# Splitting w_out only in the first tile of each MLP and fetching the split parts from DRAM afterwards

## What is computed

```
x = attention(q, k, v)           # 8 heads of 64; each row sees 96 local and 8 global keys
h = x @ w_in;  g = h * cos(h);   x = g @ w_out          # MLP 1, d_ff 2048
h = relu(x @ w_in2);             out = (h * h) @ w_out2  # MLP 2, d_ff 2048
```

## Time and profile before

| | before |
|---|---|
| device time, median of 3 | 1246.7 us |
| device time of the profiled execution | 1248.4 us |
| its span, first to last instruction | 1246.6 us |
| TensorE busy | 1218.5 us (98%) |
| DVE busy | 736.8 us (59%) |
| ACT busy | 559.6 us (45%) |
| Pool busy | 625.1 us (50%) |
| DMA packets | 118.8 MB, 32.6% of the 16 engines' time |
| granted TensorE clock | 0.999 |

### The profile page before, as it was taken

The page is one execution under the profiler, slowest core; times in us unless marked ns, Lnnn a source line. Parts: engine busy times, 40 slices in busy tenths (PEclk is TensorE's granted clock), DMA queues, the critical chain, the costliest instruction groups (busy, mean ns, idle before and its releaser), DMA issues.

```text
span 1246.6 us, 18120 instructions
## 1 busy us (share of the span) xinstructions
PE 1218.5 (98%) x6240; PEld 991.6 (80%) x6240; DVE 736.8 (59%) x1434; ACT 559.6 (45%) x1164; POOL 625.1 (50%) x687
## 2 busy tenths in 40 slices
PE   5789999999999999999999999999999999999998
PEld 3667888887888877888888888888888888888887
DVE  6579988888878888788888933223323223223222
ACT  4656767666666666676433322222222222222211
POOL 4468966555666665666543433333334334333332
PEclk9999999999999999999999999999999999999999
DMA  4523434333433333342155441131131221311211
GB/s 122 146 70 102 110 101 137 97 89 92 146 97 104 124 89 104 112 133 84 54 148 177 138 138 52 51 111 51 51 116 46 81 89 49 113 51 51 78 50 60
DMA packets 150949, 118.80 MB, mean 95 GB/s; under 512 B 63680, under 2 KB 115008, under 8 KB 150848
## 3 DMA queue, kind: packets, MB, share of 16 engines
q1 hardware_dynamic: 150848, 117.55, 32.6%
HBM read 96.54 MB, written 20.97 MB: 94 GB/s over the span
## 4 chain that ended last, share of the span: by engine, by line
PE 94%; DVE 2%; ACT 1%; POOL 1%; DMA 1%; issue 1%; SPq 0%; DVEq 0%; ACTq 0%; POOLq 0%
PE psum L557 14%; PE psum L559 14%; PE psum L558 14%; PE psum L576 8%; PE psum L582 7%; PE psum L583 7%; PE psum L581 7%; PE psum L578 7%; PE psum L577 7%; PE psum L651 3%; PE psum L615 3%; PE psum L636 2%; PE psum L593 1%; ACT probs L771 1%; POOL probs L487 0%
## 5 line engine op out<-in xcount | busy, mean ns | idle before, releaser
L472 POOL TENSOR_SCALAR w_out_hi<-w_out_raw 128x512 fp32r<-128x512 f32 x192 | 136.5, 711 | 549.8 <-PE psum L583 312.6
L557 PE MATMUL psum<-x_parts,w_in_hi 128*128 128x512 f32 x768 | 302.9, 394 | 2.6 <-ACT hs L800 2.6
L559 PE MATMUL psum<-x_parts,w_in_lo 128*128 128x512 f32 x768 | 299.4, 390 | 0.0
L558 PE MATMUL psum<-x_parts,w_in_hi 128*128 128x512 f32 x768 | 298.8, 389 | 0.0
L474 POOL TENSOR_TENSOR w_out_lo<-w_out_raw,w_out_hi 128x512 fp32r<-128x512 f32 x192 | 264.2, 1376 | 16.0
L1017 DVE TENSOR_TENSOR g_lo<-act_a,g_hi 128x512 fp32r<-128x512 f32 x192 | 139.9, 729 | 187.1 <-ACT g_hi L812 181.7
L802 ACT ACTIVATE hs<-psum 128x512 f32<-128x512 f32 x96 | 57.4, 598 | 359.9 <-PE psum L559 359.9
L557 PEld LDWEIGHTS psum<-x_parts,w_in_hi 128*128 128x128 f32 x768 | 144.2, 188 | 32.0 <-issue 3.6
L559 PEld LDWEIGHTS psum<-x_parts,w_in_lo 128*128 128x128 f32 x768 | 144.2, 188 | 30.6
L558 PEld LDWEIGHTS psum<-x_parts,w_in_hi 128*128 128x128 f32 x768 | 144.4, 188 | 28.9
L576 PE MATMUL psum<-g_hi,w_out_hi 128*128 128x512 f32 x384 | 157.7, 411 | 0.5 <-issue 0.5
(11 more groups left out here) (76 smaller groups left out, 1657.6 us busy)
## 6 DMA issues: line engine op xcount, KB each, us to landing
w_out_raw<-in_moe_w_out_dram SPq DMA_DIRECT2D x192, 256.0 KB, 2.7
vals<-in_v_dram SPq DMA_DIRECT2D x80, 112.0 KB
w_stage<-in_moe_w_in_dram SPq DMA_DIRECT2D x32, 256.0 KB, 3.0
w_dram<-w_stage SPq DMA_DIRECT2D x16, 512.0 KB, 3.3
raw<-in_k_dram SPq DMA_DIRECT2D x96, 64.0 KB, 2.5
raw<-in_q_dram SPq DMA_DIRECT2D x96, 64.0 KB, 2.3
y_dram<-y_stage SPq DMA_DIRECT2D x24, 256.0 KB, 3.7
x_raw<-y_dram SPq DMA_DIRECT2D x6, 1024.0 KB, 5.1
```

The lines of the kernel that those rows point to most:

```text
L472: pool.tensor_scalar(hi, row, 1.0, 1.0, ALU.mult, ALU.mult).then_inc(w_out_hi_ready, 1)
L557: pe.matmul(to, hi, x[:, 0, c], start=(c == 0), stop=False)
L558: pe.matmul(to, hi, x[:, 1, c], start=False, stop=False)
L559: last = pe.matmul(to, lo, x[:, 0, c], start=False, stop=(c == KC - 1))
```

## The change

The parts of `w_out` become one tensor, hi and lo side by side. Pool splits a chunk only where `is_split(F)` is true, which is in steps 0 to 15 and 96 to 111, the first tile of each MLP. SP then stores the two parts (512 KB) in the new `w_out_dram`, and in the other 160 steps fetches them from there by one DMA of 512 KB. `split_out(F)` gets one more condition: the buffer that it writes, that of step F - 3, must have been stored.

```diff
+    w_out_dram = nc.dram_tensor("w_out_dram", (2, FC, P, 2, DM), F32, kind="Internal").ap()
...
-            w_out_hi = sb("w_out_hi", [P, 3, DM], F32R, lay)
-            w_out_lo = sb("w_out_lo", [P, 3, DM], F32R, lay)
+            w_out = sb("w_out", [P, 3, 2, DM], F32R, lay)
...
+        def is_split(F):
+            return F % STEPS < FC
...
             def load_w_out(F):
-                src, f = (w1_out if F < STEPS else w2_out), F % FC
-                if F >= 2:
-                    sp.wait_ge(w_out_ready, F - 1)
+                if not is_split(F):
+                    return
+                src, f, n = (w1_out if F < STEPS else w2_out), F % FC, splits(F)
+                if n >= 2:
+                    sp.wait_ge(w_out_ready, n - 1)
                 sp.dma_start(w_out_raw[:, F % 2], src[P * f:P * f + P, :]).then_inc(w_out_loaded[F % 2], 16)
+
+            def store_w_out(F):
+                if is_split(F):
+                    sp.wait_ge(w_out_ready, splits(F) + 1)
+                    sp.dma_start(w_out_dram[F // STEPS, F % FC], w_out[:, F % 3].bitcast(F32)).then_inc(w_out_stored[F % 3], 16)
+
+            def fetch_w_out(F):
+                if F >= STEPS_ALL or is_split(F):
+                    return
+                sp.wait_ge(down_done, KC * (F - 2))
+                for s in range(3) if F % STEPS == FC else (F % 3,):
+                    sp.wait_ge(w_out_stored[s], 16 * slot_splits(F - F % 3 + s if F % 3 >= s else F - F % 3 + s - 3))
+                sp.dma_start(w_out[:, F % 3].bitcast(F32), w_out_dram[F // STEPS, F % FC]).then_inc(w_out_fetched[F % 3], 16)
...
+                store_w_out(F)
+                store_w_out(F + 1)
+                fetch_w_out(F + 2)
                 if F + 4 < STEPS_ALL:
                     load_w_out(F + 4)
                 if s == 0 and i > 0:
                     store(i - 1)
                 if F + 5 < STEPS_ALL:
                     load_w_out(F + 5)
+                fetch_w_out(F + 3)
...
             def split_out(F):
-                pool.wait_ge(w_out_loaded[F % 2], 16 * (F // 2 + 1))
+                if not is_split(F):
+                    return
+                n = splits(F)
+                pool.wait_ge(w_out_loaded[F % 2], 16 * (n // 2 + 1))
                 if F >= 3:
                     pool.wait_ge(down_done, KC * (F - 2))
+                    pool.wait_ge(w_out_stored[F % 3], 16 * slot_splits(F))
...
             def down(F, window):
                 i, f = divmod(F, FC)
-                pe.wait_ge(w_out_ready, F + 1)
+                if is_split(F):
+                    pe.wait_ge(w_out_ready, splits(F) + 1)
+                else:
+                    pe.wait_ge(w_out_fetched[F % 3], 16 * (slot_fetches(F) + 1))
```

More of the change, by code:

```diff
@@ L201, in build @@
         w_out_hi_ready = sem("w_out_hi_ready")
+        w_out_stored = [sem(f"w_out_stored{i}") for i in range(3)]
+        w_out_fetched = [sem(f"w_out_fetched{i}") for i in range(3)]
         w_out_ready = sem("w_out_ready")
@@ L234, in tails, with splits, slot_splits, slot_fetches @@
             return sum(place(n)[1] > 0 for n in range(G + 1))
+        def is_split(F):
+            return F % STEPS < FC
+        def splits(F):
+            return sum(is_split(n) for n in range(F))
+        def slot_splits(F):
+            return sum(is_split(n) for n in range(F % 3, F, 3))
+        def slot_fetches(F):
+            return sum(not is_split(n) for n in range(F % 3, F, 3))
         def x_lo_wait(eng, i, window):
@@ L467, in split_out @@
             def split_out(F):
-                pool.wait_ge(w_out_loaded[F % 2], 16 * (F // 2 + 1))
+                if not is_split(F):
+                    return
+                n = splits(F)
+                pool.wait_ge(w_out_loaded[F % 2], 16 * (n // 2 + 1))
                 if F >= 3:
                     pool.wait_ge(down_done, KC * (F - 2))
-                row, hi, lo = w_out_raw[:, F % 2], w_out_hi[:, F % 3], w_out_lo[:, F % 3]
+                    pool.wait_ge(w_out_stored[F % 3], 16 * slot_splits(F))
+                row, hi, lo = w_out_raw[:, F % 2], w_out[:, F % 3, 0], w_out[:, F % 3, 1]
                 pool.tensor_scalar(hi, row, 1.0, 1.0, ALU.mult, ALU.mult).then_inc(w_out_hi_ready, 1)
-                pool.wait_ge(w_out_hi_ready, F + 1)
+                pool.wait_ge(w_out_hi_ready, n + 1)
                 pool.tensor_tensor(lo, row, hi.bitcast(F32), ALU.subtract).then_inc(w_out_ready, 1)
@@ L574, in down @@
                     if i < TILES:
-                        hi, lo = w_out_hi[:, F % 3, cols], w_out_lo[:, F % 3, cols]
+                        hi, lo = w_out[:, F % 3, 0, cols], w_out[:, F % 3, 1, cols]
                         pe.matmul(to, hi, g_hi[:, F % 3], start=one, stop=False)
@@ L580, in down @@
                         hi, lo = g_hi[:, F % 3, cols], g_lo[:, F % 3, cols]
-                        pe.matmul(to, hi, w_out_hi[:, F % 3], start=one, stop=False)
-                        pe.matmul(to, hi, w_out_lo[:, F % 3], start=False, stop=False)
-                        last = pe.matmul(to, lo, w_out_hi[:, F % 3], start=False, stop=end)
+                        pe.matmul(to, hi, w_out[:, F % 3, 0], start=one, stop=False)
+                        pe.matmul(to, hi, w_out[:, F % 3, 1], start=False, stop=False)
+                        last = pe.matmul(to, lo, w_out[:, F % 3, 0], start=False, stop=end)
                     last.then_inc(down_done, 1)
```

## The result

The changed kernel takes 1252.84 us (median of 8 executions, 1251.20 to 1253.59), the kernel before 1248.49 us in the same runs (median of 8, 1246.59 to 1251.14). The ratio is 1.0032, with a 95% interval of 1.0023 to 1.0041: 4.0 us slower (0.32%), between 2.9 and 5.1. The forecast was 1254.0 us, against a median of 1246.7 that three executions had shown; as a difference, 7.3 us was forecast and about 4 came. Slower was right, the size was too large by some 3 us. (The two medians of eight are 4.35 us apart; the ratio puts the difference at 4.0.) That 1252.84 lies only 1.2 us under the forecast of 1254.0 is partly luck: the forecast started from 1246.7, which is 1.8 us under the later median of 1248.49, and this hides more than half of the error in the size.

A forecast was written before the change was run, and what follows sets the result against it. After the prologue TensorE works without a gap and bounds the kernel. Removal 0, later tiles 0 and first-tile loop 7.3 us, added to the runs' 1246.7, give 1254.0 us; range 1248 to 1261.

The forecast's parts named there:

- Removal at 0: Later tiles: taking 160 splits, 334 us, from Pool gains 0 us, since TensorE waits for nobody there.
- Fetches at 0: Later tiles: 160 fetches of 512 KB, each landing in 3.3 to 5.1 us, cost 0 with 8 us to spare.
- The first fetch: Step 16, pair 7: waits for all stores, taking 10 of the pair's 13.9 us; cost 0, bound 1 or 2 us.
- The loop: First tile: store, Pool's splits and normalise, SP's `load_w_in`; 16.3 us a turn against 13.9; 7.3 us lost, chance 0.62.
- SP's return path: First tile: SP's `load_w_in` waits for Pool's `split_in`, so the next store leaves late; about 4.1 us a turn.
- The rival without a stall: First tile: Pool's instructions take their shorter whole-span means, a turn is 14.95 us; 1.3 us lost, 1248.0 us, chance 0.22.
- the one of stores landing in pairs: First tile: both stores land together at 5.1 us, adding 7.2 us, to 1261 us; much slower, chance 0.12.
- The last link: Pair 4: late `move_tail(16)` delays `copy_qk(16)`, then `front(12)`, which `up(13)` needs; second stall, 3.9 us.
- store, start of issue to landing: First tile, each turn: 0.4 us to issue and 3.3 us to land, 3.7 us; four such latencies in the chain.
- stall at `up(12)`: Pair 3: TensorE waits for Pool's late `split_in(12)`; first stall, 1.2 us.
- The stall at `up(15)`: Pair 4 to 5: TensorE waits for `front(14)`, late behind `move_tail(17)`; third stall, 2.2 us, 7.3 in all.
- signs of being wrong: No new TensorE idle time before 170 us, store landings off 3.3 us, or `down` waiting for `w_out_fetched` in later tiles.

The follow-up runs named there:

- Second tile: Against the changed kernel: Pool splits `w_out` in the first two tiles of each MLP, parts stored in the second, fetched in the other four; 1248.69 us.
- stores first: Against the changed kernel: the two stores of a pair moved to the head of SP's pair, ahead of the loads of queries, keys and values; 1248.72 us.
- Stores only: Against the changed kernel: Pool splits `w_out` in all tiles and nothing is fetched; first-tile stores and the waits for them stay; 1252.82 us.
- third stage: Against the changed kernel: three staging buffers for `w_in` instead of two, so SP's `load_w_in` waits for the split before last; 1249.68 us.
- swapped: Against the changed kernel: the two stores of a pair in the other order, so the one `split_out(F+3)` needs goes second; 1255.78 us.
- the run made to cut it: Against the changed kernel: in pairs 4 and 5 ACT does `front` ahead of `copy_qk`; 1252.24 us, ratio 1.0036 to the kernel before.

## Why the prediction was right, and where its size was off

**Removal at 0: right.** Second tile takes 293 us from Pool and gains nothing; with the stores first, 374 us. **Fetches at 0: right.** Stores only has no fetch and loses as much as the changed kernel, stores first has all of them and loses nothing. The first fetch, which I held for the tightest, made nobody wait. A fetch lands after 3.6 us, within the 3.3 to 5.1 us.

**The loop: right in each of its links up to Pool's lateness**, by its cuts: the store's place (stores first), SP's return path (third stage), Pool's `split_in` in the same pairs (second tile), and the store's landing (swapped). The rival without a stall, and the one of stores landing in pairs, did not come. The last link, from Pool over `move_tail`, `copy_qk` and `front` to `up(13)`, is what the chain shows; the run made to cut it changed more than that link.

**The size: 7.3 us forecast, 4.0 measured.** The profiled execution runs 0.56 us later than that of before already at `up(5)` (91.54 against 90.98), ahead of the stretch in question, and 0.57 us at `up(12)` (141.83 against 141.26), where nothing has been lost yet; I take 0.57 off below. Lateness against before, in us:

| term | forecast | profile after | worked out from |
|---|---|---|---|
| store, start of issue to landing | 3.7 | 2.72, 2.74, 3.69 | the chain |
| `split_in(8)` | 1.4 | 0.2 | 107.76 + 1.61 - 108.55 - 0.57 |
| `split_in(12)` | 5.8 | 2.8 | 140.01 - 136.66 - 0.57 |
| `move_tail(16)` | 6.1 | 2.6 | 145.12 - 141.92 - 0.57 |
| `copy_qk(16)` to the end of `front(12)` | 4.5 | 5.6 | 150.81 - 145.21 |
| stall at `up(12)` | 1.2 | 0 | |
| start of `up(13)` | 5.1 | 2.9 | 150.96 - 147.50 - 0.57 |
| start of `up(15)` | 7.3 | 4.5 | 166.68 - 161.57 - 0.57 |

*The step that was mis-sized is the store.* I counted the column "us to landing" from the end of the issue and added 0.4 us for the issue. The chain counts from the start of the issue, and the first store of a pair landed 2.7 us after it in two of three turns, a whole microsecond less than my 3.7. The median of the page, 4.2 us, is one over both stores of a pair; in pairs 1 and 2 the shorter of the two is 2.7 and the longer 4.2 us. That I multiplied by four shows in the sum: 1.0, 1.0, 0.0 and (pair 4, landed after 2.8 us) 0.9, or 2.9 us. The fit of 3.2 us that the prediction cites beside it from the Trainium skill ("DMA: Bandwidth & Descriptors", section "Anatomy of one DMA") is for transfers that GpSimd issues, and here SP issues them; the sum does not rest on it.

*A smaller part was Pool.* In pair 3 `normalise` took 2.77 us and `split_in(12)` 1.98 us, in place of 3.6 and 2.45: 1.3 us less. This fits the mechanism of the rival without a stall, Pool running against another part of DVE's list, but no run shows that this is the reason. Of the 3.0 us by which `split_in(12)` is less late than forecast, the stores are 1.9 and Pool 1.3, and SP's way from `split_in(10)` to the store takes back 0.5 (124.38 to 128.93 is 4.55 us, in place of 4.1); the rest are terms of 0.3 us and less.

*In the other direction* two things were missing. The way from `copy_qk(16)` to `front(12)` was 1.1 us longer, because the gate on DVE took 2.40 in place of 1.31 us and ACT waited for it. And the half clock behind the stall cost 1.45 us in this execution: from `up(13)` to `scores(16)` TensorE took 155.22 - 150.96 = 4.26 us, where it took 2.81 before. With it 2.9 becomes 4.4, and another 0.1 to 0.2 us lie ahead of `up(15)`.

*The stall at `up(15)`* is not there in the first profile of the changed kernel, but it is 1.5 us in its second one and in stores only. In which waits the 4 us come is thus not the same in each execution; their sum nearly is.

How much of the 4 us is the clock? The executions in which the mean granted clock was 1.0 (to three digits) show the kernels with hardly any half clock: 1251.20 and 1250.54 us for the changed kernel, which has only these two, and a median of 1247.01 for 20 of the kernel before. That is 3.5 to 4.2 us of waiting. As far as two executions show it, the half clock adds a spread to both kernels and little to the difference.

*Smaller misses.* The prediction put Pool's busy time near 290 us and it is 248: the normalisations, which are the same 192 in both kernels, took 95.2 in place of 128.0 us. A landing off 3.3 us stood among its signs of being wrong, and it came, though as a shorter one for the store that counts. Three stores in a row come to 3.3 + 1.8 + 1.8 = 6.9 us by its own rows, and not to "about 6"; nothing hung on it.

## What to carry to other kernels

Work taken from an engine is worth something only where another engine waits for it; a share of busy time over the whole program hides the one stretch that counts, and the change added its wait just there. A wait for a DMA in an engine's list is to be priced as a loop: which queue issues that DMA, what does that queue wait for, and does this come back to the same engine; if a turn is longer than the rhythm, the lateness grows until something breaks. The cure that cost nothing was to issue the store as early in its queue as its data allow.

## What was unexpected of the hardware

The time of one execution goes with the mean granted clock of its core, in steps. Of 63 executions of the kernel before, the 20 with a clock of 1.0 have a median of 1247.01 us, the 26 with 0.999 have 1248.65, the 10 with 0.997 have 1250.30, and the 7 with 0.996 have 1251.56. A mean lower by 0.004 over 1247 us is 5 us of full-speed work, near the 4.5 us between the first and the last of these medians. So this spread goes with stretches of TensorE at 1.2 GHz and is not mere noise; a difference of 0.3% is best read between executions of the same clock. The three times shown of the kernel before, with a median of 1246.7, happened to hold two of the fastest.

Pool's relief shortened DVE's work: its 1434 instructions take 670 us in the changed kernel, 669 with the stores first, and 737 in both kernels in which Pool splits all tiles (before and stores only). The Trainium skill ("SBUF — State Buffer", section "Who interferes with whom") has a DVE instruction with two inputs in SBUF and a GpSimd instruction that reads SBUF exclude each other; these 67 us agree with it, though no run shows single instructions excluding each other. They are no use here, since DVE's full stretch is the first tile, in which Pool's work is the same.
